# The first batch's gates stored from SP's queue, between two weight pieces, instead of from ACT's queue

## The reference

```python
def reference(q, k, v, moe_w_in, moe_w_out, moe2_expert_emb, moe2_tau, moe2_w1, moe2_w2):
    # 1. attention: 4 x 8 heads, 576 tokens, 64 wide, causal window of 128, ALiBi bias
    x = attention(q, k, v).reshape(2304, 512)
    # 2. MLP: 512 -> 2048 -> 512
    h = x @ w_in
    x = (h * np.clip(h + 3.0, 0.0, 6.0) / 6.0) @ w_out
    # 3. eight experts, top 1: 512 -> 1024 -> 512
    xn = x / (norm(x) + 1e-6);  en = expert_emb / (norm(expert_emb) + 1e-6)
    logits = xn @ en.T / tau
    expert_idx = np.argmax(logits, axis=1)
    gate_w = softmax(logits)[arange, expert_idx]
    for e in range(8):
        mask = expert_idx == e
        out[mask] = gate_w[mask, None] * (np.maximum(x[mask] @ w1[e], 0) @ w2[e])
    return out
```

## Time and profile before

| | us |
|---|---|
| median of 3 runs | 838.8 |
| lowest and highest run | 838.38, 839.31 |
| the profiled execution's own time | 838.55 |
| its span in the profile | 836.8 |
| mean granted TensorE clock | 0.997 of full |
| busy: PE, DVE, ACT, POOL | 823.3, 477.9, 395.8, 241.5 |

### The profile page before, as it was taken

One profiled execution on the slowest core, in us unless ns is written; L12 is line 12 of the kernel. 1 busy time (PEld: TensorE's weight loads), 2 busy tenths in 40 slices (PEclk: granted clock), 3 DMA queues, 4 the chain that ended last, 5 costly groups with the idle time before them and its releaser, 6 DMA issues.

```text
span 836.8 us, 18599 instructions
## 1 busy us (share of the span) xinstructions
PE 823.3 (98%) x6533; PEld 707.0 (84%) x6533; DVE 477.9 (57%) x1469; ACT 395.8 (47%) x1057; POOL 241.5 (29%) x261
## 2 busy tenths in 40 slices
PE   7999999999999999999999999999999999999996
PEld 6888888888888888888888888888888888888885
DVE  7765575665766656756565578776543445554000
ACT  5674555545455455554554337533434334343442
POOL 5992000000000000000000101386665656666432
PEclk9999999999999999999999999999999999999999
DMA  8764211102112111121100026575555444552100
GB/s 243 226 190 152 77 52 58 33 15 76 52 41 69 33 40 51 52 76 35 32 13 2 27 88 168 167 224 176 165 161 169 128 140 140 164 157 66 50 14 11
DMA packets 54427, 80.18 MB, mean 96 GB/s; under 512 B 11752, under 2 KB 28136, under 8 KB 54210
## 3 DMA queue, kind: packets, MB, share of 16 engines
q1 hardware_dynamic: 47986, 67.57, 26.6%
q0 software_dynamic: 4000, 11.29, 4.2%
q10 hardware_dynamic: 2352, 0.14, 0.3%
HBM read 69.51 MB, written 11.30 MB: 97 GB/s over the span
## 4 chain that ended last, share of the span: by engine, by line
PE 94%; DMA 2%; DVE 2%; issue 0%; ACT 0%; SPq 0%; POOL 0%; POOLq 0%; ACTq 0%; DVEq 0%
PE ps_h L852 24%; PE ps_y L869 22%; PE ps_h L1004 16%; PE ps_s L1033 15%; PE ps_out L797 4%; PE ps_s L755 3%; PE ps_y L1028 3%; PE ps_out L1033 1%; PE ps_out L956 1%; DMA y_scratch<-gate_tok 1%; PE ps_s L774 1%; DMA arena<-in_k 1%; PE ps_s L780 1%; PE ps_s L777 1%; DMA en_all<-y_scratch,gather_ids 0%
## 5 line engine op out<-in xcount | busy, mean ns | idle before, releaser
L852 PE MATMUL ps_h<-x_hi,win_hi 128*128 128x256 f32 x576 | 165.6, 295 | 0.1
L852 PE MATMUL ps_h<-x_lo,win_hi 128*128 128x256 f32 x576 | 158.5, 283 | 0.0
L852 PE MATMUL ps_h<-x_hi,win_lo 128*128 128x256 f32 x576 | 158.3, 283 | 0.0
L1160 ACT CAST gated_hi<-gated 128x256 fp32r<-128x256 f32 x144 | 58.5, 406 | 138.3 <-PE ps_y L869 98.4
L1428 DVE TENSOR_TENSOR gated_lo<-gated,gated_hi 128x256 fp32r<-128x256 f32 x144 | 64.6, 449 | 101.9 <-ACT gated_hi L1160 101.9
L852 PEld LDWEIGHTS ps_h<-x_hi,win_hi 128*128 128x128 f32 x576 | 107.8, 190 | 8.3 <-issue 2.7
L869 PE MATMUL ps_y<-wout_hi,gated_hi 128*128 128x512 f32 x288 | 114.1, 396 | 0.0
L869 PE MATMUL ps_y<-wout_hi,gated_lo 128*128 128x512 f32 x288 | 113.8, 395 | 0.0
L628 POOL MEMSET arena<- 128x64 bf16 x2 | 0.2, 151 | 390.8 <-DVE x_lo L1402 390.8
L869 PE MATMUL ps_y<-wout_lo,gated_hi 128*128 128x512 f32 x288 | 112.1, 389 | 0.0
L852 PEld LDWEIGHTS ps_h<-x_hi,win_lo 128*128 128x128 f32 x576 | 107.9, 191 | 2.3
(11 more groups left out here) (241 smaller groups left out, 1563.7 us busy)
## 6 DMA issues: line engine op xcount, KB each, us to landing
arena<-in_moe_w SPq DMA_DIRECT2D x64, 512.0 KB, 4.2
arena<-in_v SPq DMA_DIRECT2D x40, 128.0 KB, 3.2
y_scratch<-y_sb SPq DMA_DIRECT2D x9, 512.0 KB, 3.8
en_all<-in_moe_w_in SPq DMA_DIRECT2D x16, 256.0 KB, 3.9
arena<-in_v SPq DMA_DIRECT2D x16, 256.0 KB, 3.2
en_all<-in_moe_w_out SPq DMA_DIRECT2D x16, 256.0 KB, 3.9
arena<-in_q SPq DMA_DIRECT2D x31, 128.0 KB, 2.4
arena<-in_k SPq DMA_DIRECT2D x31, 128.0 KB, 2.9
```

The costliest lines, as they stand in the source:

```text
L852: last = pe.matmul(ps_h[m % 2][:, 0:TB], a[:, c, w], r[:, c, x], start=n == 0, stop=n == 3 * KC - 1)
L1160: act.copy(gh[m % 2][:], gate[:]).then_inc(act_gh, 1)
```

## The change

The gates of the first batch are stored by SP, between its DMAs for the second and the third piece of the first expert's weights, after a wait for `dve_gate`. ACT no longer waits for `dve_gate` in slot 10 and issues no store. The store itself (`store_gates` with tiles 0 to 15) stays as it is, as does all else.

```diff
@@ -560,6 +560,10 @@
             sp.wait_ge(dve_order, 2)
             e = expert_of(0)
             for n in range(RAWS):
+                if n == 2:
+
+                    sp.wait_ge(dve_gate, 1)
+                    store_gates(sp, 0, EARLY_TILES)
                 load_piece(n, e)
             for n in range(RAWS, 2 * NC):
                 load_piece(n, e)
@@ -1171,10 +1175,6 @@
                     root(1)
                 if f == 7:
                     gate_exp(0)
-                if f == 10:
-
-                    act.wait_ge(dve_gate, 1)
-                    store_gates(act, 0, EARLY_TILES)
                 if 10 <= f <= FC + 1:
                     first_expert(f - 10)
```

## The result

| | before | after |
|---|---|---|
| median of 6 runs | 838.78 us | 842.48 us |
| lowest and highest run | 838.19, 839.31 | 841.41, 842.88 |
| profiled execution, its span | 838.55, 836.8 | 842.41, 840.6 |
| ratio to the kernel before | | 1.0043, interval [1.003, 1.0056] |

The change makes the kernel 3.7 us slower. That is 1.5 us above the end of the predicted range, on the side of rival B.

What follows compares the result with a forecast made beforehand. PE, busy 98% of the span, was taken as the bound. From 838.55 us, 0.57 for the gather's wait went off and 1.0 for late piece 2 came on: 839.0, range 837.8 to 841.0.

Steps and rivals of the forecast that it cites:

- rival B: Weights behind the store on SP's queue lengthen it to 10.34 us; piece 2 lands 3.9 us late; 841.0 us, chance 0.18.
- The bound and the gain: PE bounds the kernel; its wait for the first gather, 0.57 us, goes entirely.
- ACT's part at nothing: ACT loses one wait and one DMA issue in slot 10; nothing waits for it there, so no gain.
- SP's issue at 501.0: SP, already waiting, issues the gates' store at about 501.0 where ACT issued at 501.26: a gain of 0.3 us.
- The store's landing: The first batch's gates land in DRAM at 509.6, from 501.0 + 1.0 + 4.9 + 2.7; bounds 503.7 and 511.35.
- Part 1: From the store's issue until its small packets run: shrinks from 2.7 us to the 1.0 us of an empty queue.
- part 2: The stretch in which the store's small packets run: 4.9 us, as before, some engines standing long in a 4-byte write.
- part 3: From the store's last busy slice to its landing: 2.7 us, as before.
- piece 2's landing: First expert's weight piece 2, behind the store on SP's queue, lands at about 509.4, 1.9 us after ACT wants it.
- The slack of 0.9 us: Of piece 2's lateness, 0.48 us before DVE's cast and 0.4 before PE's last down product are free.
- Rival C: No effect: small packets wait their 2.7 us whatever the queue, gates land at 511.35, piece 2 on time; 838.3 us, chance 0.07.

Runs made afterwards that it cites:

- e13: Kernel before without the gates' store; SP instead writes 2048 constant values into the same column at 470.6. 838.37 us against 839.12.
- e16: Kernel before, but gates of tiles 0 to 13 computed and stored early (483.5), square root's table loaded ahead, tiles 14 and 15 stored in slot 10. 838.37 us, ratio 0.9989.
- e14: e13, with SP also waiting for the gates between pieces 1 and 2, so pieces 2 to 4 leave late. 838.59 us, ratio 0.999.
- e7: Kernel before with the gates' store on SP's queue behind piece 4, all five pieces issued as early as before. 843.72 us, ratio 1.0005.
- e2: Changed kernel, but SP waits for the store's landing before issuing piece 2, so the store runs alone. 845.0 us, ratio 1.0022.
- e1: Kernel before with the store still on ACT's queue, but SP waits for the gates between pieces 1 and 2. 847.52 us, ratio 1.0039.
- e5: Kernel before, unchanged, traced on another chip. 843.26 us, ratio 0.9999.
- e4: Changed kernel with the store one piece later, between pieces 2 and 3. 840.92 us against 843.33 for the kernel before, ratio 0.998.
- e3: Changed kernel, but pieces 2 to 4 are issued right after SP's wait and the store behind them, same queue. 846.35 us, ratio 1.0048.
- e10: e3 plus a store between pieces 1 and 2: the same 8 KB as 2048 separate values, packed in a DRAM array of its own. 855.02 us, ratio 1.0188.
- e15: Changed kernel with the store between pieces 3 and 4, in a repeated set of runs. 838.75 us, ratio 0.9998.
- e6: The changed kernel, unchanged, run again on another chip. 843.8 us, ratio 1.0017.

## Why the prediction was wrong

*The bound and the gain* held. PE's wait for the gather was the only thing to win: it went, and e13 and e16 show the kernel without it at 0.1% less (e14, with 0.3 us of it left, too).

*ACT's part at nothing* (e7, in which only the queue differs: 1.0005) and *SP's issue at 501.0* (measured 501.16) held.

*The store's landing*: forecast 509.6, measured 510.9. Part 1 was right (first packets 1.0 us after the issue). The sum of parts 2 and 3 was nearly right (7.6, measured 8.7), but what I made of them was not. I had taken part 2 for a few engines standing in a write, and part 3 for a tail that comes when the last of them is through. That is how the trace of before looks, where the store's last packets start at 508.9; it does not carry over. In e2 the writes leave the engines in 2 us and need 7 more to be finished.

*The step that failed* is piece 2's landing: forecast 509.4, measured 512.14. From the reading of part 2 I concluded that an engine which is through with its small packets moves weights at full pace, 8 packets in 1.5 us. In the trace of before nothing new wanted to move in that stretch: the packets of pieces 0 to 4 had all started by 505.3, and piece 5 left at 509.43. The 10 GB/s of the earlier trace rows could mean "nothing to do" or "nothing can be done", and I took the first. The windows of the changed kernel (16 to 131 GB/s) and e1 say the second. The term of the sum: late by 4.5 us (512.2 against 507.7) instead of 1.9. If piece 2 can't be reported before the store, the store's landing at 510.9 makes 1.5 of the 2.7 us by which it came later than forecast, and the weights' pace the other 1.2; that the pace alone would do it is not excluded.

One sign of it was in the trace of before, and the earlier trace rows hid it. The 6.5 us there is the longest of 13 pieces, not of all 64: the view counts a piece only where the record of its landings is complete. Piece 4, issued at 497.62, landed whole at 509.66, after 12.0 us (8.5 in e13, with no small write near). e5's trace of the same kernel is complete enough to list its piece 4:

```profile
DMA to landing us min/median/max: 3.4/4.6/12.6
```

Nobody waits for piece 4 before 513.9, so it cost nothing there.

*The slack of 0.9 us* held. Late by 4.5 less 0.9 is 3.6; the last down product should start at 517.32 + 3.6 and the 0.2 us by which this trace is behind already at 495: 521.1. It starts at 521.00:

```profile
521.00 0.50 PE L873 MATMUL ps_y<-wout_hi,gated_hi 128*128 128x512 f32 x1 [0.26 <-DVE gated_lo L1428]
...
522.97 0.70 PE L1008 MATMUL ps_h<-win_hi,x_hi 128*128 128x512 f32 x2 [0.34 <-issue]
```

The second line is a term that was missing. The first expert product starts 3.6 us later than before (519.36), not 3.1, since PE now reaches it 0.34 us before it may start; by the order of the code and ACT's timeline (x_hi copied from 522.29 to 522.86, behind two splits of pieces) it waits for ACT. Together: 838.55 - 0.57 + 3.6 + 0.5 + 0.2 = 842.3; the profiled run has 842.41.

*Rival B* had the right sign and place, and a wrong mechanism: it let the weights behind the store lengthen it (e2: they don't; in e1, where both ran at once from two queues, the store did take 16.60 us), where the store holds up the weights. Its 10.34 us for the store was dearer than the truth, and its landing of piece 2, "at about 511.4", still too early, since it too had the piece follow at once.

*The Trainium skill's* section (Queues, rings and completion order of "DMA: Bandwidth & Descriptors") has two rules on this. The first, that a completion lands only after every earlier write of its engine, fits wherever piece 2 stood behind the small writes: it was never reported before the gates' landing. But that can't be all that holds piece 2: in e4 and e1 it stood ahead of the small writes and was held too. By the first rule alone the prediction had the loss at 0.6 us; what neither the rule nor my sum had is that loads crawl for as long as the landing of 2048 small writes is outstanding. The second, that an engine takes turns between the rings, fits e1 in part: 1060 small packets and 66 of the weights' ran side by side from 504 to 505, but the small ones had started only 2.8 us after their issue (503.8), and why, no run shows. *Rival C* is out: in the changed kernel the small packets started 1.0 us after the issue.

## What to carry to other kernels

Count the separate writes of a store, not its bytes: 8 KB in 2048 writes of 4 bytes took 9.7 us and held up the loads beside and behind it, 8 KB in 128 runs took 1.6 us and held up nothing. Put such a store where nothing is being loaded (e16). Behind the loads that are needed first it spares them, but comes late itself (e3); another queue is no protection (e1). And when a trace shows DMA engines idle or standing, ask what was waiting to move: a stretch in which nothing was asked for says nothing about what could have been had.

## What the runs showed of the hardware

- After 2048 stores of 4 bytes to DRAM had left the DMA engines (2 us), their completion took until 9.7 us after the issue, on empty engines (e2). In the meantime loads in 4 KB packets moved at 16 to 131 GB/s instead of some 300 (changed kernel, 504 to 510). Whether the DRAM or the path to it is what is busy, no run tells.
- Loads that stood ahead of such a store were held too: in the kernel before piece 4 landed after 12.0 us (8.5 in e13), and in e4 one of the 16 engines' shares of piece 2 landed 7.9 us after the other 15.
- Packed values were not faster than values 2052 bytes apart (e10: 11.5 us, with pieces behind them; the gates' own, with pieces behind them, 8.9 in e15 to 10.8 in e6).
- Behind a wait of PE of 3.1 us the granted clock went to 1.2 GHz for some 3.5 us and made a late gather dearer by 1.6 us (e5); behind one of 3.2 us it stayed at 2.4 GHz (e7). In the changed kernel PE's waits came in pieces, the longest 1.4 us in the first trace and 2.0 in e6, and in neither did the clock fall there.
- Executions and chips differ in this store: in the kernel before it landed after 10.3 us in the trace from one chip and 11.8 in the trace from another (e5), and the kernel's median was 838.8 us on the first and 843.2 on the second.
